# Attention ahead of two expert layers: batch 0's outputs scaled later, strided tokens grouped modulo 8, V loaded in one transfer, idle matmuls around the q and k transposes

## The chip, the cores and the metric

The program runs on one core of a Trainium2 chip. The metric is the device time of one execution in microseconds. TensorE (PE) does matmuls and transposes, VectorE (DVE), ScalarE (ACT) and GpSimd (POOL) do elementwise work, and SyncE (SP) issues the transfers. ACT issues some too. All engines run their own instruction streams and meet only at semaphores.

## What is computed

```
# q, k, v: 4 batches x 8 heads x 576 tokens x 64
scores = q @ k.T / 8
mask_local   = (rel >= 0) & (rel < 32)               # heads 0 to 3
mask_strided = (rel >= 0) & (pos_k % 32 == pos_q % 32)   # heads 4 to 7
attn = softmax(where(mask, scores, -1e9)) @ v        # -> x, 2304 tokens x 512
h = x @ w_in;  g = h * sigmoid(1.702 h);  x = g @ w_out          # d_ff 2048
# top 2 of 8 experts, d_ff 1024, noisy gate
out[token] += weight * (relu(x @ w1[e]) @ w2[e])
```

## The kernel before

**Three stages.** Stage A is the attention, stage B the dense layer with the splitting of the experts' weights beside it, stage D the experts. The change is to stage A and the head of the program, up to about 190 us.

**Stage A.** The eight heads of a batch make four pairs `hp` (0 and 1 local, 2 and 3 strided), so there are 16 pairs `i = 4 b + hp`. The PE program has a prologue (transposes of q and k and the scores of pairs 0 and 1) and then one *body* for each pair. Body `i` holds, in this order: `transpose_p` of head 0 of pair `i`, `transpose_qk` for q and for k of pair `i+2`, `p_times_v` of head 0, `transpose_p` of head 1, `scores` of pair `i+2` head 0, `p_times_v` of head 1, `scores` of pair `i+2` head 1. In the last two bodies the parts of pair `i+2` are replaced by first matmuls of stage B (`mlp_ahead`). Below, T(i) is the time at which the q transposes of body `i` start. The order is written out by hand; nothing is scheduled by a tool.

**Who feeds whom.** `ps_t` (two banks) takes all transposes, and ACT copies them out (`evac_pt`, `evac_qk`). DVE takes row maxima of the scores and subtracts them (`max_and_sub`), ACT takes the exponential (`exps`), DVE sums (`sums`), POOL normalises (`norm`), and PE transposes the result. The output of a pair stands in `ps_o`. ACT writes its scaled fp16 high part (`out_hi`) and DVE the remainder (`out_lo`) into `x1`.

**Scales.** V, w_in, the gate weights and w_out each get one power-of-two factor from their absolute maximum. DVE takes maxima over pieces (`v_max`, `weights_max`, by `absmax`), then the piece results are joined and `raw_max` is counted up. PE spreads the joined column over the partitions by one small matmul that stands at the head of a `scores` (argument `spread`, with a wait on `raw_max`). DVE reduces that (`ALL_OF`), and `power_of_two` makes the factor in five short steps. ACT and DVE then split w_in in eighths in four bodies from `SPLIT_IN`, and w_out from `SPLIT_OUT`.

**Loads.** SP issues them in program order: `load_qk` four transfers with rows of 64 numbers, `load_v` five for a local pair and eight for a strided one, `v_flat` two transfers of 2.3 MB over all of V for its maximum. A strided pair's 576 tokens are treated as 8 groups of 72: with token = 32 j + 4 g + r, group g has the tokens of all j and r.

**Idle matmuls.** `busy` issues matmuls on constants that nobody reads: 12 of 512 columns ahead of the first data, and 4 of 224 columns ahead of each `p_times_v`.

Of the kernel before, what the change touches and what calls it, by code (L numbers as in the profile page):

```python
# [68 lines left out]
MAX_IN, SPLIT_IN, MAX_OUT, SPLIT_OUT = 1, 6, 9, 14  # L69
assert (MAX_IN + QUARTERS) % 4 == 1 and (MAX_OUT + QUARTERS) % 4 == 1  # L70
# [6 lines left out]
def program(nc, q, k, v, w_in, w_out, w_gate, w_noise, noise, w1, w2, out):  # L77
    ctx = ExitStack()
    with ctx:
# [188 lines left out]
        def w2_of(par, part, f):  # L268
# [24 lines left out]
            "consts_pool busy_set qk_in0 qk_in1 v_in0 v_in1 v_in2 v_in3 v_flat_in0 v_flat_in1 w_in_in w_out_in "  # L293
            "small_in t_done t_evac s_done mx_done sub_done exp_done sum_done rr_done norm_done pv_done "
            "x1_hi x1_lo raw_max scaled step split_hi split_lo "
# [18 lines left out]

        def is_local(hp):
            return hp < PAIRS // 2

        V_DMAS = [5, 5, 2 * SRES, 2 * SRES]
# [18 lines left out]
        def out_views(b, hp, part):  # L337

            tok = slice(b * SEQ, (b + 1) * SEQ) if isinstance(b, int) else bass.ds(b * SEQ, SEQ)
            dst = x1[:, part, hp, tok]  # L340
# [48 lines left out]
        def _(sp):  # L389
# [12 lines left out]

            load_qk(0, 0)
            load_qk(0, 1)

            sp.dma_start(w_in_s[:].rearrange("p a c f -> p (a c f)").bitcast(F32)[:, 0:HEADS * SEQ],
                         v[0:2].rearrange("b h (x s) d -> (b h x) (s d)", x=P // (2 * HEADS))
                         ).then_inc(S["v_flat_in0"], 16)
            sp.dma_start(w_out_s[:].rearrange("p a c f -> p (a c f)").bitcast(F32)[:, 0:HEADS * SEQ],
                         v[2:4].rearrange("b h (x s) d -> (b h x) (s d)", x=P // (2 * HEADS))  # L410
                         ).then_inc(S["v_flat_in1"], 16)
            load_v(sp, 0, 0)
            load_v(sp, 0, 1)
# [4 lines left out]
            for i in range(NPAIR - 2):  # L418

                sp.wait_ge(S["s_done"], i * 2 + 2)  # L420
                load_qk((i + 2) // PAIRS, (i + 2) % PAIRS)
                load_v(sp, (i + 2) // PAIRS, (i + 2) % PAIRS)
                if i < QUARTERS:
                    c = DC // QUARTERS
                    wait(sp, S["w_in_in"], 16 * i)
                    sp.dma_start(w_in_raw[:, i * c:(i + 1) * c], w_in.rearrange("(c p) f -> p c f", p=P)[:, i * c:(i + 1) * c]
                                 ).then_inc(S["w_in_in"], 16)
                n, c = i - SPLIT_IN - 3, FC // QUARTERS
# [284 lines left out]
        def _(act):  # L713
            def evac_qk(n, hp, which):
# [26 lines left out]
            def out_hi(b, hp):  # L741
                i = b * PAIRS + hp
                act.wait_ge(S["pv_done"], i * 2 + 2)
                if i == 0:
# [221 lines left out]
        def _(dve):  # L966
# [11 lines left out]
            def power_of_two(src, scale, inverse, link):  # L978
# [11 lines left out]
            v_flat = [t[:].rearrange("p a c f -> p (a c f)").bitcast(F32)[:, 0:HEADS * SEQ]  # L990
                      for t in (w_in_s, w_out_s)]
# [25 lines left out]
            def out_lo(b, hp):  # L1017
                i = b * PAIRS + hp
                dve.wait_ge(S["x1_hi"], i + 1)
                for (src, hi), (_, lo) in zip(out_views(b, hp, 0), out_views(b, hp, 1)):  # L1020
                    last_op = nc.vector.scalar_tensor_tensor(lo, src, col(S_V), hi, ALU.mult, ALU.subtract)  # L1021
                last_op.then_inc(S["x1_lo"], 1)

            def v_max(n):

                half = HEADS * SEQ // 2
                dve.wait_ge(S[f"v_flat_in{n // 2}"], 16)
# [3 lines left out]
            max_and_sub(0, 0, 0)  # L1031
            max_and_sub(0, 0, 1)
            v_max(0)
            sums(0, 0, 0)
            sums(0, 0, 1)
            v_max(1)
            max_and_sub(0, 1, 0)
            max_and_sub(0, 1, 1)
            v_max(2)
# [11 lines left out]
            ALL_OF = {0: V_ALL, 1: WG_ALL, MAX_IN + QUARTERS: WI_ALL, MAX_OUT + QUARTERS: WO_ALL}  # L1051
# [20 lines left out]
            def weights(i):  # L1072

                if i == 0:
                    dve.wait_ge(S["small_in"], 48)
                    nc.vector.tensor_reduce(col(B_MAX), wg[:], AX.XY, ALU.max, apply_absolute_value=True
                                            ).then_inc(S["raw_max"], 1)
                if MAX_IN <= i < MAX_IN + QUARTERS:
                    weights_max(S["w_in_in"], i - MAX_IN)
                if i == SPLIT_IN - 1:  # L1080
                    dve.wait_ge(S["all_max"], 3)
                    power_of_two(col(WI_ALL), col(S_WI), col(I_WI), step).then_inc(S["scaled"], 1)
                if i == 2 * PAIRS:
                    dve.sem_inc(S["raw_max"], 1)
                if MAX_OUT <= i < MAX_OUT + QUARTERS:
                    weights_max(S["w_out_in"], i - MAX_OUT)
# [11 lines left out]
            def stage_a(b, last=False):  # L1098
                for hp in range(PAIRS):
# [7 lines left out]
                    if i == 0:  # L1107
                        v_max(3)
# [767 lines left out]
```

## Time and profile before

| | |
|---|---|
| median of 3 runs | 1030.38 us (1029.64 to 1032.16) |
| the profiled execution | 1028.2 us |
| its span, first to last instruction | 1026.4 us |
| PE busy | 978.1 us (95% of the span) |
| DVE, ACT, POOL busy | 594.5, 307.6, 219.8 us |
| mean granted TensorE clock | 0.976 |

The profile is of one execution, so sums that are made with its rows stand against 1028.2 us; what they give is then put on the median. A busy share is a mean over stages with different limits. "Granted clock" 1.00 is 2.4 GHz and 0.50 is 1.2 GHz.

### The profile page before, as it was taken

What the parts mean: (1) busy time and instruction counts of PE and PEld (TensorE: products, weight loads), DVE (VectorE), ACT (ScalarE), POOL (GpSimd) and SP (SyncE); (2) the same over time, 40 slices, a digit from 0 to 9 for tenths busy, and PEclk for the clock granted to TensorE, in tenths of its full rate; (3) what the DMA queues carried; (4) which work ended last, traced back from release to release, by engine and by line L of the source; (5) the groups of instructions that cost most, each with busy time, mean ns of one, the idle gap of its engine ahead of it and who ended that gap; (6) DMA issues with size and microseconds to landing.
All of it is one profiled execution on the core that took longest, in us unless ns stands there. A gap on an engine that the chain in (4) does not pass through costs nothing.

```text
span 1026.4 us, 22946 instructions
## 1 busy us (share of the span) xinstructions
PE 978.1 (95%) x9218; PEld 706.8 (69%) x9219; DVE 594.5 (58%) x1033; ACT 307.6 (30%) x427; POOL 219.8 (21%) x274
## 2 busy tenths in 40 slices
PE   7899999999999999999999899989999999999992
PEld 4677777867677576775765767756777767677771
DVE  6588998668777786787887744232232323233231
ACT  2355745523243233332531321111111111111110
POOL 4222323000000000010025124233323333333331
PEclk8699999999999999999999999999999999999997
DMA  9774582097756667567647635848474747475330
GB/s 267 177 187 92 129 196 55 6 393 237 249 204 205 247 214 258 181 205 268 219 149 238 218 78 151 263 114 213 131 210 121 221 120 214 133 209 142 89 82 23
DMA packets 170240, 182.43 MB, mean 178 GB/s; under 512 B 133495, under 2 KB 133495, under 8 KB 167360
## 3 DMA queue, kind: packets, MB, share of 16 engines
q1 hardware_dynamic: 112832, 142.47, 44.6%
q0 software_dynamic: 9600, 27.69, 8.9%
q10 hardware_dynamic: 47744, 11.35, 6.3%
q8 instruction: 48, 0.79, 0.3%
q14 instruction: 16, 0.13, 0.0%
HBM read 116.41 MB, written 53.55 MB: 166 GB/s over the span
## 4 chain that ended last, share of the span: by engine, by line
PE 86%; DVE 4%; DMA 2%; SPq 2%; ACT 2%; issue 1%; POOLq 0%; DVEq 0%; ACTq 0%
PE bank L1760 20%; PE bank L1769 20%; PE bank L1661 18%; PE bank L1586 17%; PE bank L1524 4%; PE bank L1562 3%; PE bank L1494 2%; PE bank L1536 1%; PE bank L1543 1%; PE bank L1513 1%; DMA arena<-out,arena 1%; DMA arena<-in_moe_w 1%; DVE sc L976 1%; SPq L399 1%; ACT arena L725 1%
## 5 line engine op out<-in xcount | busy, mean ns | idle before, releaser
L1586 PE MATMUL bank<-x,w_in_s 128*128 128x256 f16 (+1 forms) x1728 | 194.1, 273 | 2.6 <-DVE x L1021 1.5
L1661 PE MATMUL bank<-w_out_s,arena 128*128 128x512 f16 x864 | 190.2, 379 | 0.0
L1586 PEld LDWEIGHTS bank<-x,w_in_s 128*128 128x128 f16 x1728 | 167.9, 98 | 25.9 <-DVE x L1021 1.8
L1661 PEld LDWEIGHTS bank<-w_out_s,arena 128*128 128x128 f16 x864 | 83.6, 98 | 96.6
L1429 DVE TENSOR_TENSOR arena<-arena 128x512 f32<-128x512 f32 x37 | 25.6, 692 | 161.7 <-ACT arena L899 117.6
L1760 PEld LDWEIGHTS bank<-arena,w_out_s 128*128 128x128 f16 x2016 | 114.5, 98 | 5.9 <-issue 0.8
L1760 PE MATMUL bank<-arena,w_out_s 128*128 128x128 f16 x2016 | 117.0, 219 | 0.6 <-issue 0.6
L1760 PEld LDWEIGHTS bank<-arena,w_in_s 128*128 128x128 f16 x1920 | 109.3, 98 | 5.4 <-issue 0.7
L1760 PE MATMUL bank<-arena,w_in_s 128*128 128x128 f16 x1920 | 111.7, 219 | 0.5 <-issue 0.5
L1769 PE MATMUL bank<-w_out_s,arena 128*128 128x512 f16 x480 | 108.7, 383 | 3.3 <-DVE arena L1424 3.3
L1769 PE MATMUL bank<-w_in_s,arena 128*128 128x512 f16 x480 | 108.6, 383 | 2.3 <-DVE arena L1424 2.3
L1422 DVE CAST arena<-arena 128x512 f16<-128x512 f32 x82 | 35.5, 433 | 124.0 <-ACT arena L894 113.2
L976 DVE TENSOR_REDUCE sc<-arena 128x1 f32<-128x512 f32 (+2 forms) x42 | 100.4, 2404 | 7.6 <-DMA arena<-in_moe_w 4.0
L894 ACT ACTIVATE arena<-bank 128x512 f32<-128x512 f32 x82 | 48.9, 597 | 167.4 <-PE bank L1760 152.3
L1158 DVE SCALAR_TENSOR_TENSOR arena<-arena,sc 128x4096 f16<-128x4096 f32 x16 | 71.7, 4483 | 34.7 <-ACT arena L803 34.7
L1769 PEld LDWEIGHTS bank<-w_out_s,arena 128*128 128x128 f16 x480 | 46.5, 99 | 56.7 <-issue 5.9
L1769 PEld LDWEIGHTS bank<-w_in_s,arena 128*128 128x128 f16 x480 | 46.5, 99 | 55.8 <-issue 2.8
L899 ACT ACTIVATE arena<-bank,arena 128x512 f32<-128x512 f32 x40 | 27.5, 687 | 185.9 <-PE bank L1769 182.7
L803 ACT ACTIVATE arena<-arena,sc 128x4096 f16<-128x4096 f32 x16 | 59.3, 3709 | 61.9 <-DVE sc L985 61.9
L632 POOL DMA_INDIRECT arena<-out,arena x37 | 44.2, 1196 | 130.7 <-DMA out<-arena 116.6
L565 POOL TENSOR_TENSOR arena<-arena 96x768 f32<-96x768 f32 (+1 forms) x32 | 44.2, 1397 | 124.8 <-DVE arena L1015 124.7
L637 POOL DMA_INDIRECT out<-arena x40 | 41.4, 1034 | 104.5 <-DVE arena L1429 98.4
(196 smaller groups left out, 992.8 us busy)
## 6 DMA issues: line engine op xcount, KB each, us to landing
arena<-in_moe_w SPq DMA_DIRECT2D x16, 2048.0 KB, 11.5
split_weights<-arena SPq DMA_DIRECT2D x16, 2048.0 KB, 7.4
w_in_s<-split_weights SPq DMA_DIRECT2D x32, 512.0 KB
w_out_s<-split_weights SPq DMA_DIRECT2D x32, 512.0 KB
arena<-in_q SPq DMA_DIRECT2D x32, 144.0 KB, 3.6
arena<-in_k SPq DMA_DIRECT2D x32, 144.0 KB, 3.7
out<-zeros SPq DMA_DIRECT2D x1, 4608.0 KB, 25.1
x_rows<-arena SPq DMA_DIRECT2D x18, 256.0 KB, 3.3
```

The costliest lines, as they stand in the source:

```text
L565: pool.tensor_tensor(pr, pr, rr[hp % 2][0:nq, h2, 0:nb].unsqueeze(2).to_broadcast([nq, nb, nk]), ALU.mult).then_inc(S["norm_done"], 1)
L632: pool.indirect_dma_start(out=prior[b4 % 2], out_offset=None, in_=out, in_offset=bass.IndirectOffsetOnAxis(ap=cur[b4], axis=0), bounds_che ...
L637: pool.indirect_dma_start(out=out, out_offset=bass.IndirectOffsetOnAxis(ap=cur[b4], axis=0), in_=ysb[b4 % 2], in_offset=None, bounds_check ...
L803: nc.scalar.activation(halves[:, 0], raw[m], ACT.Copy, scale=col(S_U + m)).then_inc(S["unit_hi"], 1)
L894: nc.scalar.activation(hf[half], ps_dh[half], ACT.Relu, scale=DOWN).then_inc(S["relu_done"], 1)
L976: return nc.vector.tensor_reduce(dst, src, AX.X, ALU.max, apply_absolute_value=True)
L1158: nc.vector.scalar_tensor_tensor(halves[:, 1], raw[m], col(S_U + m), halves[:, 0], ALU.mult, ALU.subtract).then_inc(S["unit_lo"], 1)
L1524: last = mm(dst, ql, kr, start=False, stop=True, skip_group_check=True)
L1586: last = mm(dst, w_in_s[:, w_part, c, f * P:(f + 1) * P], x1[:, x_part, c, tok], start=(c == 0 and w_part + x_part == 0), stop=(c == DC - ...
L1661: last = mm(ps_x[j], g[par][:, g_part, f, j * P:(j + 1) * P], w_out_s[:, w_part, f], start=(n == 0), stop=(n == 3 * FC - 1))
L1760: last = mm(ps_dh[half][:, n * P:(n + 1) * P], w1_of(w_par, w_part, c, f), xt[par][:, x_part * DC + c], start=(c == 0 and w_part + x_part ...
L1769: last = mm(ps_y[par], h[par][:, h_part, f * P:(f + 1) * P], w2_of(w_par, w_part, f), start=(n == 0), stop=(n == 3 * EFC - 1))
```

## The change

- **Loads.** `load_qk` of pair 2 is issued once the transposes of pair 0 are done, that of pair 3 after those of pair 1. The loads of all of V for its maximum come in four parts of 1.2 MB between them. `load_v` of pairs 0 and 1 is issued by ACT. A strided pair's V comes in one transfer, with rows of 512 numbers.
- **Groups.** token = 8 p + n, group n has all p. So `evac_qk`, the output of `p_times_v` and `out_views` have other access patterns: q and k are written one number at a time with 72 numbers from one to the next, where before four lay side by side; `p_times_v` writes every fourth number of the bank, where before it wrote four side by side out of sixteen.
- **Batch 0's outputs.** ACT copies them unscaled as fp32 into a free part of `x1` (`held_out`). In batch 1 each body has one more scaling on ACT and one more remainder on DVE for them.
- **Maxima.** They move to other bodies. The last pieces of w_in and w_out are now taken inside bodies 6 and 13, ahead of the spreading matmul of the same body (before: at the end of bodies 4 and 12).
- **Idle matmuls.** Two or four of 512 columns between the steps of the prologue, one of 256 columns ahead of each half of `transpose_qk` in the bodies (into a score bank, with a new wait on `sub_done`), and none now ahead of `p_times_v` of head 0.

```diff
-MAX_IN, SPLIT_IN, MAX_OUT, SPLIT_OUT = 1, 6, 9, 14
+SPLIT_IN, SPLIT_OUT = 7, 14
...
+        held_out = [x1[:, 0, hp, 2 * SEQ:4 * SEQ].bitcast(F32) for hp in range(PAIRS)]
...
-        V_DMAS = [5, 5, 2 * SRES, 2 * SRES]
+        V_DMAS = [5, 5, 1, 1]
...
-            dst = dst.rearrange("p (j a x) -> p a j x", j=SLEN, a=2)
-            src = ps_o[:, :, 0:SEQ // 2].rearrange("p a (j x) -> p a j x", j=SLEN)
+            dst = dst.rearrange("p (k a n) -> p a k n", k=SQ, a=2)
+            src = ps_o[:, :, 0:SEQ // 2].rearrange("p a (k n) -> p a k n", k=SQ)
...
-                s = s.rearrange("h (j g r) d -> h r j g d", j=SLEN, g=SB)
-                for h2 in range(2):
-                    for r in range(SRES):
-                        eng.dma_start(vn[hp][r:SQ:SRES, :, h2], s[h2, r]).then_inc(v_in[hp], 16)
+                eng.dma_start(v_tile(hp)[0:SQ].rearrange("p h n d -> p h (n d)"),
+                              s.rearrange("h (p n) d -> p h (n d)", n=SB)).then_inc(v_in[hp], 16)
...
+            sp.wait_ge(S["t_done"], 4)
+            load_qk(0, 2)
+            load_v_flat(0)
+            sp.wait_ge(S["t_done"], 8)
+            load_qk(0, 3)
+            load_v_flat(1)
...
# ACT
-                    dst = dst.rearrange("c (g a j r) -> c a j g r", g=SB, a=2, j=SLEN // 2)
-                    src = src.rearrange("c a (j g r) -> c a j g r", g=SB, r=SRES)
+                    dst = dst.rearrange("c (n a p) -> c a p n", n=SB, a=2)
+                    src = src.rearrange("c a (p n) -> c a p n", n=SB)
...
+                if b == 1:
+                    act.wait_ge(S["x1_lo"], 2 + hp)
+                    nc.scalar.activation(x1[:, 0, hp, 0:SEQ], held_out[hp], ACT.Copy, scale=col(S_V)
+                                         ).then_inc(S["late_hi"], 1)
...
             evac_qk(1, 0, 1)
+            load_v(act, 0, 0)
...
             exps(0, 0, 1)
+            load_v(act, 0, 1)
# DVE
-            ALL_OF = {0: V_ALL, 1: WG_ALL, MAX_IN + QUARTERS: WI_ALL, MAX_OUT + QUARTERS: WO_ALL}
+            ALL_OF = {PAIRS: V_ALL, SPLIT_IN - 1: WI_ALL, 2 * PAIRS + 2: WG_ALL, SPLIT_OUT - 1: WO_ALL}
...
+                    if i == SPLIT_IN - 1:
+                        weights_max(S["w_in_in"], QUARTERS - 1)
+                    if i == SPLIT_OUT - 1:
+                        weights_max(S["w_out_in"], QUARTERS - 1)
                     weights_lo(i, 0)
# PE
+                    busy(idle, slice(0, 2 * P), ps_s[0][:, 0])
                     wait(pe, S["t_evac"], n * 2 + a - 1)
...
-                busy(4, slice(SEQ // 2, 4 * P))
+                if h2 == 1:
+                    busy(4, slice(SEQ // 2, 4 * P))
...
-                        o = o.rearrange("p (j n r) -> p n j r", j=SLEN, n=half)[:, m % half]
+                        o = o.rearrange("p (k n) -> p n k", n=half)[:, m % half]
...
+                    spread = (V_MAX, b + 2) if hp == 0 and not last else (B_MAX, 2 * b + 2) if hp == 2 else None
+                    if hp == 1 and last:
+                        spread = (B_MAX, 7)
...
+                        pe.wait_ge(S["sub_done"], i * 2 + 3)
+                        transpose_qk(k[1], hp2, 0, loads, 1)
+                        transpose_qk(k[2], hp2, 1, loads, 1)
```

The first place is SP's queue at the head of the program, from the load of all of V on. Before, ten transfers of V stand ahead of q and k of pair 2:

```order
L406 DMA w_in_s<-in_v 128x4608
L409 DMA w_out_s<-in_v 128x4608
L351 DMA arena<-in_v 128x2x64
L356 DMA arena<-in_v 32x5x64
L357 DMA arena<-in_v 96x5x64
L356 DMA arena<-in_v 32x5x64
L357 DMA arena<-in_v 96x5x64
L351 DMA arena<-in_v 128x2x64
```

Now pair 2 stands right behind the first eight loads of q and k (here from the third line on), and the V of a strided pair is one row (the last but one):

```order
L402 DMA arena<-in_q 96x6x64 x2
L402 DMA arena<-in_k 96x6x64 x2
L402 DMA arena<-in_q 96x6x64 x2
L402 DMA arena<-in_k 96x6x64 x2
L410 DMA w_in_s<-in_v 128x2304
L402 DMA arena<-in_q 96x6x64 x2
L402 DMA arena<-in_k 96x6x64 x2
L410 DMA w_in_s<-in_v 128x2304
...
L402 DMA arena<-in_k 96x6x64 x2
L366 DMA arena<-in_v 72x2x512 x2
L410 DMA w_out_s<-in_v 128x2304
```

So q and k of pairs 2 and 3 have moved ahead of V, and V's maximum takes its data in between.

The second place is DVE around the last piece of w_in. Before, the piece and the joining of the four results end body 4, and the sums of body 5 and its maxima follow. (`L976` is `absmax`, `L1013` the sums, `L998` the score maxima, `L1000` the reduction of the spread column.)

```order
L976 TENSOR_REDUCE sc<-arena 128x1
L976 TENSOR_REDUCE sc<-sc 128x1
L1013 TENSOR_REDUCE arena<-arena 72x8
L1015 RECIPROCAL arena<-arena 72x8
L1013 TENSOR_REDUCE arena<-arena 72x8
L1015 RECIPROCAL arena<-arena 72x8
L998 TENSOR_REDUCE arena<-bank 72x8
L1000 TENSOR_REDUCE sc<-bank 128x1
```

Now, at the turn from body 5 to body 6 (`L999` is `absmax`, `L1037` the sums, `L1022` the score maxima, `L1024` the reduction of the spread column):

```order
L999 TENSOR_REDUCE sc<-arena 128x1 [waits w_in_in]
L1037 TENSOR_REDUCE arena<-arena 72x8 [waits exp_done]
L1039 RECIPROCAL arena<-arena 72x8 [waits sum_done]
L1037 TENSOR_REDUCE arena<-arena 72x8 [waits exp_done]
L1039 RECIPROCAL arena<-arena 72x8 [waits sum_done]
L999 TENSOR_REDUCE sc<-arena 128x1 [waits w_in_in]
L999 TENSOR_REDUCE sc<-sc 128x1 [waits step]
L1022 TENSOR_REDUCE arena<-bank 96x6 [waits s_done]
L1024 TENSOR_REDUCE sc<-bank 128x1
```

The third piece ends body 5, and the fourth with the joining stands behind the sums of body 6. Body 13 has the same rows for w_out.

## Rows read from the trace of the kernel before

**Rows 1.** The page: granted clock, 40 slices of the span, in tenths.

```profile
PEclk8699999999999999999999999999999999999997
```

**Rows 2.** Timeline of the first 45 us: start, length, engine, line, what [idle before].

```profile
10.32 0.53 PE L1513 MATMUL bank<-arena,identb 96*96 96x384 bf16 x2
12.26 0.71 PE L1494 MATMUL bank<-ident,arena 96*128 96x96 f32 x6
...
28.71 2.46 PE L1494 MATMUL bank<-ident,arena 96*128 96x96 f32 x12 [6.56 <-DMA arena<-in_k]
...
36.40 0.27 PE L1508 MATMUL bank<-identb,sc 128*128 128x128 bf16 x1 [1.21 <-DVE sc L976]
...
40.84 0.14 DVE L980 TENSOR_SCALAR sc<-sc 128x1 f32<-128x1 f32 x1
...
41.59 0.15 DVE L985 TENSOR_SCALAR sc<-sc 128x1 f32<-128x1 f32 x1
...
42.80 1.28 PE L1524 MATMUL bank<-arena 64*72 64x72 f32 x16
...
44.97 0.30 PE L1494 MATMUL bank<-ident,arena 96*128 96x96 f32 x1 [0.25 <-ACT arena L732]
```

**Rows 3.** Timeline of the same stretch, SP's queue.

```profile
11.47 5.91 SPq L351 DMA_DIRECT2D arena<-in_v  x1
...
25.13 1.06 SPq L399 DMA_DIRECT2D arena<-in_k  x2
```

**Rows 4.** Windows of 1 us: PE, PEld, DVE, ACT, POOL busy, granted clock, DMA share, GB/s.

```profile
15.00:16.00 1.00, 1.00 (x8) 0.99 (x8) 1.00 (x1) 0.96 (x2) 0.00 (x0) 0.78 0.90 387
...
42.00:43.00 1.00, 1.00 (x6) 0.40 (x5) 0.00 (x0) 0.72 (x1) 0.00 (x0) 0.56 0.17 38
```

**Rows 5.** Timeline, PE in bodies 7 and 8 (body 8 has body 0's shapes).

```profile
105.79 1.21 PE L1562 MATMUL bank<-arena 72*64 72x72 f32 x16
...
113.90 0.77 PE L1494 MATMUL bank<-ident,arena 96*128 96x96 f32 x6 [0.25 <-ACT arena L732]
114.87 0.77 PE L1494 MATMUL bank<-ident,arena 96*128 96x96 f32 x6 [0.20 <-ACT arena L725]
115.48 0.55 PE L1543 MATMUL bank<-busy_in 128*128 128x224 bf16 x4
115.95 1.21 PE L1562 MATMUL bank<-arena 128*64 128x96 f32 x12
...
117.64 0.22 PE L1508 MATMUL bank<-identb,sc 128*128 128x128 bf16 x1
...
121.22 1.25 PE L1524 MATMUL bank<-arena 64*72 64x72 f32 x16
...
123.37 0.77 PE L1494 MATMUL bank<-ident,arena 96*128 96x96 f32 x6 [0.25 <-ACT arena L732]
```

**Rows 6.** Timeline, end of body 12 and body 13 (starts 162.7 us).

```profile
160.22 0.74 ACT L747 ACTIVATE x<-bank,sc 128x576 f16<-128x576 f32 x1 [2.65 <-PE bank L1562]
...
162.16 0.71 ACT L732 ACTIVATE arena<-bank 128x288 f32<-128x288 f32 x2 [1.21 <-PE bank L1536]
...
163.23 2.27 DVE L976 TENSOR_REDUCE sc<-arena 128x1 f32<-128x2048 f32 x1
...
165.54 0.16 DVE L976 TENSOR_REDUCE sc<-sc 128x1 f32<-128x4 f32 x1
...
166.44 0.22 PE L1508 MATMUL bank<-identb,sc 128*128 128x128 bf16 x1
...
167.24 0.20 DVE L1015 RECIPROCAL arena<-arena 72x8 f32<-72x8 f32 x1
```

**Rows 7.** Timeline of PE behind a wait in stage D.

```profile
670.49 7.03 PE L1769 MATMUL bank<-w_out_s,arena 128*128 128x512 f16 x24 [3.28 <-DVE arena L1424]
```

**Rows 8.** The window of half a microsecond behind it, columns as in rows 4.

```profile
671.00:671.50 0.50, 0.50 (x3) 0.22 (x2) 0.47 (x2) 0.00 (x0) 0.12 (x1) 0.50 0.45 85
```

**Rows 9.** Timeline of the start of stage B, matmuls of 512 columns at full clock.

```profile
208.92 6.64 PE L1661 MATMUL bank<-w_out_s,arena 128*128 128x512 f16 x30
```

More of the change, by code:

```diff
@@ L401, in load_qk, with load_v_flat @@
                                      ).then_inc(qk_in[par], 16)
+            def load_v_flat(n):
+                half = HEADS * SEQ // 2
+                at = slice(n % 2 * half, (n % 2 + 1) * half)
+                rows = v[n // 2 * 2:n // 2 * 2 + 2].rearrange("b h (x s) d -> (b h x) (s d)", x=P // (2 * HEADS))
+                sp.dma_start(v_flat[n // 2][:, at], rows[:, at]).then_inc(S[f"v_flat_in{n}"], 16)
             load_qk(0, 0)
             load_qk(0, 1)
[L406 to L413, printed above, removed]
+            sp.wait_ge(S["t_done"], 4)
[4 more added lines that the diff above has]
+            load_v_flat(1)
             sp.dma_start(wg[:, :, 0:E], w_gate.rearrange("(c p) e -> p c e", p=P)).then_inc(S["small_in"], 16)
@@ L416, in _ @@
             sp.dma_start(noise_sb[:], noise.rearrange("(t p) e -> p t e", p=P)).then_inc(S["small_in"], 16)
-            for i in range(NPAIR - 2):
-                sp.wait_ge(S["s_done"], i * 2 + 2)
+            for i in range(2, NPAIR - 2):
+                sp.wait_ge(S["t_done"], 8 * i - 2)
                 load_qk((i + 2) // PAIRS, (i + 2) % PAIRS)
+                if i == 2:
+                    load_v(sp, 0, 2)
+                    load_v(sp, 0, 3)
+                if i <= 3:
+                    load_v_flat(i)
+                sp.wait_ge(S["pv_done"], 2 * i - 2)
                 load_v(sp, (i + 2) // PAIRS, (i + 2) % PAIRS)
-                if i < QUARTERS:
+                for n in ([0], [1], [2, 3])[i - 2] if i < 5 else []:
                     c = DC // QUARTERS
-                    wait(sp, S["w_in_in"], 16 * i)
-                    sp.dma_start(w_in_raw[:, i * c:(i + 1) * c], w_in.rearrange("(c p) f -> p c f", p=P)[:, i * c:(i + 1) * c]
+                    wait(sp, S["w_in_in"], 16 * n)
+                    sp.dma_start(w_in_raw[:, n * c:(n + 1) * c], w_in.rearrange("(c p) f -> p c f", p=P)[:, n * c:(n + 1) * c]
                                  ).then_inc(S["w_in_in"], 16)
-                n, c = i - SPLIT_IN - 3, FC // QUARTERS
+                n, c = i - SPLIT_IN - 1, FC // QUARTERS
                 if 0 <= n < QUARTERS:
@@ L743, in out_hi @@
                 act.wait_ge(S["pv_done"], i * 2 + 2)
-                if i == 0:
+                if b == 0:
+                    for src, dst in out_views(b, hp, None):
+                        last_op = nc.scalar.activation(dst, src, ACT.Copy)
+                    last_op.then_inc(S["x1_lo"], 1)
+                    return
+                if i == PAIRS:
                     act.wait_ge(S["scaled"], 1)
@@ L1072, in weights @@
             def weights(i):
[L1074 to L1079, printed above, removed]
+                if i < 3:
+                    v_max(i + 1)
+                if i == 2:
+                    dve.wait_ge(S["step"], steps[0])
+                    absmax(col(V_MAX), col(PART_MAX, 4)).then_inc(S["raw_max"], 1)
+                if 3 <= i < SPLIT_IN - 1:
+                    weights_max(S["w_in_in"], i - 3)
+                if i == SPLIT_IN:
+                    gate_max()
                 if i == SPLIT_IN - 1:
-                    dve.wait_ge(S["all_max"], 3)
+                    dve.wait_ge(S["all_max"], 2)
                     power_of_two(col(WI_ALL), col(S_WI), col(I_WI), step).then_inc(S["scaled"], 1)
[L1083 to L1086, printed above, removed]
+                if SPLIT_IN + 3 <= i < SPLIT_OUT - 1:
+                    weights_max(S["w_out_in"], i - SPLIT_IN - 3)
                 if i == SPLIT_OUT - 1:
@@ L1107, in stage_a @@
                     if i == 0:
[L1108 to L1110 removed]
+                        v_max(0)
+                    if i == SPLIT_IN - 1:
+                        weights_max(S["w_in_in"], QUARTERS - 1)
+                    if i == SPLIT_OUT - 1:
+                        weights_max(S["w_out_in"], QUARTERS - 1)
                     weights_lo(i, 0)
@@ L1485, in _, with busy, transpose_qk @@
             mm = nc.tensor.matmul
-            def transpose_qk(n, hp, which, loads):
+            def busy(n, columns=slice(0, 4 * P), ps=ps_busy):
+                for _ in range(n):
+                    mm(ps[:, columns], busy_in[:, 0:P], busy_in[:, P:P + columns.stop - columns.start],
+                       start=True, stop=True, skip_group_check=True)
+            def transpose_qk(n, hp, which, loads, idle=0):
                 pe.wait_ge(qk_in[hp % 2], loads)
@@ L1538, in transpose_p @@
                     last.then_inc(S["t_done"], 1)
-            def busy(n, columns=slice(0, 4 * P)):
-                for _ in range(n):
-                    mm(ps_busy[:, columns], busy_in[:, 0:P], busy_in[:, P:P + columns.stop - columns.start],
-                       start=True, stop=True, skip_group_check=True)
             def p_times_v(n, b, hp, h2, v_use):
@@ L1560, in p_times_v @@
                     else:
-                        o = o.rearrange("p (j n r) -> p n j r", j=SLEN, n=half)[:, m % half]
-                    last = mm(o, vn[hp][0:nk, m, h2], pt[0:nk, m * nq:(m + 1) * nq], start=True, stop=True)
+                        o = o.rearrange("p (k n) -> p n k", n=half)[:, m % half]
+                    values = vn[hp][0:nk, m, h2] if is_local(hp) else v_tile(hp)[0:nk, h2, m]
+                    last = mm(o, values, pt[0:nk, m * nq:(m + 1) * nq], start=True, stop=True)
                 last.then_inc(S["pv_done"], 1)
@@ L1569, in _ @@
             transpose_qk(1, 0, 1, 16 * QK_DMAS)
+            busy(2)
             pe.wait_ge(S["consts_pool"], 10)
             scores(0, 0, 0, 2)
+            busy(2)
             scores(0, 0, 1, 2)
+            busy(2)
             transpose_qk(2, 1, 0, 16 * QK_DMAS)
             transpose_qk(3, 1, 1, 16 * QK_DMAS)
+            busy(2)
             scores(0, 1, 0, 4)
+            busy(2)
             scores(0, 1, 1, 4)
+            busy(4)
             pe.wait_ge(S["consts_pool"], CONSTS)
@@ L1624, in stage_a @@
                     if more:
-                        scores(b2, hp2, 0, k[2] + 1,
-                               (V_MAX, 1) if hp == 0 else (B_MAX, b + 2) if hp == 1 else None)
+                        scores(b2, hp2, 0, k[2] + 1, spread)
                     else:
```

54 lines of the change are left out of this document (29 added, 25 removed).

## The prediction

> **What bounds the kernel now.** I read the page first. TensorE is busy for 95% of the span, and its granted clock is at full nearly everywhere; the exception the change can reach is the dip at the very start [rows 1]. So two questions matter: what PE waits for in the first 45 us, and what it executes or waits for in each body of stage A.
>
> The head, by the timeline: after the prologue and the first transposes of P, PE stands idle for 6.56 us until k of pair 2 has landed, and starts body 0 at 28.71 [rows 2]. The queue of SP tells why: k of pair 2 is issued only at 25.13, since one issue of the transfers of V ahead of it took 5.91 us [rows 3]. The clock had already halved at about 15.5 us and comes back only at about 42.9 [rows 4], so body 0 runs cold and takes 44.97 - 28.71 = 16.26 us [rows 2]. Body 8 has the same shapes and takes 123.37 - 113.90 = 9.47 us at full clock [rows 5].
>
> In the steady bodies PE goes from one piece to the next with only two visible gaps of 0.25 and 0.20 us around the transposes of q and k [rows 5]. DVE also has little air where weights are split, but what ends last is PE.
>
> **The change, part by part.** Gains are negative.
>
> *The head.* Q and k of pair 2 are issued once pair 0 is transposed, some 15 us earlier, so the data is there when PE arrives. What is then the path is PE's own prologue, with idle matmuls added. A group of local scores takes 12.26 - 10.32 = 1.94 us, 512 columns at full clock take 6.64 / 30 = 0.22 us [rows 2, 9]. From the end of the first group at 10.32: 0.43 idle, 1.94 scores, 0.43 idle give 13.1; the twelve transposes with their waits 115.48 - 113.90 = 1.6 [rows 5], then 0.43, 1.94, 0.43, 1.94 and 0.86 give 20.3; the six transposes of P (0.77, as six in rows 5) and the gap of 0.25 give T(0) = 21.4 against 28.71. DVE's sums lose the reduction of V that stood before them, so the normalised P does not delay this. If the clock holds, body 0 takes 9.47 less the 0.41 worked out below, so T(1) = 30.5 against 44.97: **-14.5 us**. It is also the part with the cold body in it, so the clock matters: every window of the new prologue holds 512-column matmuls where the old one had transposes with pauses, and I take it that the clock holds. ACT's own issue of V costs nothing here if its ten issues take about half a microsecond each; they stand ahead of evacuations that PE needs only later.
>
> *Idle matmuls in the bodies.* The four ahead of `p_times_v` of head 0 cost PE 115.95 - 115.48 = 0.47 us [rows 5] and nothing else is waited for there, since P was copied out before the k transposes. The new four of 256 columns take about 0.11 each. Two lie inside the gaps of 0.25 and 0.20; two stand where there is only about 0.05 of gap, and about 0.06 in all comes out behind the last. Bounds: nothing, and all 0.44. So -0.41 in each of bodies 1 to 13, **-5.3 us**, and -0.47 in bodies 14 and 15, which have no q and k: **-0.9 us**.
>
> *The moved wait.* `sub_done` is now needed before the q transposes instead of before the scores. It is for the subtraction of the body before, finished more than a microsecond earlier; nothing, unless DVE is over a microsecond late.
>
> *Batch 0's scaling.* Four copies more on ACT and four remainders more on DVE. Between the start of the output copy and the next evacuation ACT has 162.16 - 160.22 = 1.94 us, of which the copy takes 0.74 [rows 6]; a second of 0.74 fits. In body 4 it does not fit: V's factor is made there, in five steps of 40.84 to 41.74, 0.90 us [rows 2], and `out_hi` waits for them with the evacuation of the next P queued behind it. DVE is also later by a maximum of 2.27 us. **+0.7 us** (0 to 2).
>
> *The last pieces of w_in and w_out.* This is the cost that the change brings. PE's spreading matmul now waits for a maximum that stands behind both sums of the same body. In body 13 of the trace DVE does one piece from 163.23 (2.27 us) and has the sums done at 167.44; PE passes the spread at 166.44 [rows 6]. With the next piece behind the sums: 167.3 + 2.27 + 0.16 [rows 6] and a tenth from there to PE give 169.8, where PE arrives at 166.44 - 0.41 = 166.0. That is 3.8 us of idle PE. DVE comes late into both bodies: in bodies 4 and 5 for the added remainders and pieces, in 10 to 12 because pieces of w_out meet the last eighths of w_in. The bounds are 3.2 (sums limited only by the exponentials) and 5.5; I take 4.5 for each of bodies 6 and 13: **+9.0 us**.
>
> *The clock behind these stalls.* After an idle time of 3.28 us in stage D the clock stood at half [rows 7, 8]. From the spread to the first matmul of the second group of scores a cold body took 42.80 - 36.40 = 6.40 us, a warm one 121.22 - 117.64 = 3.58 [rows 2, 5], and the clock was back right there. So a stall costs another 2.8 us, twice **+5.6 us**. Bounds: nothing, and double, if it stays cold as long as it did from body 0 on.
>
> *Strided groups.* SP has seven issues fewer per strided pair; that queue is hidden behind the bodies. The access patterns are the open point. Sixteen matmuls of 72 columns that write four numbers side by side take 1.21 us, as long as twelve of 96 columns that write plainly [rows 5], so that scatter is free; no row shows single numbers. I take nothing, and up to 1.2 us per head for a doubled write. The Trainium skill speaks against the change here ("SBUF — State Buffer", section "Door 1: The DMA port swizzle"): it says that PSUM has lines of 8 bytes and SBUF of 16, that each new line costs, and that scattered PSUM access slows matmuls clearly. By that rule the old groups of four already paid in PSUM, which the equal 1.21 us speaks against.
>
> *Sum.* -14.5 - 5.3 - 0.9 + 0.7 + 9.0 + 5.6 = -5.4 us. The profiled execution took 1028.2, so 1022.8 for it; the median of the runs shown is 2.2 us above it, so **1025.0 us**.
>
> **The rivals.**
>
> 1. *The stalls stay warm.* One of 3.8 us falls so that the clock holds, or it comes back at once. For it: PE idled 1.21 us ahead of the spread in body 0, and the clock rose 6.5 us later without any change of load. Against it: 3.28 us were enough [rows 7, 8]. Time: 1025.0 - 5.6 = 1019.4.
> 2. *The prologue goes cold as before.* Small fp32 matmuls filled it and still the clock fell at 15.5 with PE almost fully busy [rows 4]. If it also falls now, some 12 us of work at half clock, by the ratio 6.40 to 3.58, take 5.3 us more: 1030.3, no change to be measured.
> 3. *Single-number writes cost.* If `p_times_v` of a strided pair doubles, 16 groups at 1.2 us give +19 and 1044; from 0.52 us per group on (8.5 us in all) the kernel is slower by over 0.3%. The rule of the Trainium skill named above ("SBUF — State Buffer") would have it so. ACT's scattered writes of q and k (a line each, where four shared one) would come on top: the k transposes wait for them.
> 4. *ACT blocks on its issues.* The mechanism is SP's 5.91 us for one issue [rows 3]. ACT issues V of pair 1 between the exponentials and the evacuation of P(0); there the new path has about 1.5 us to spare. One such issue costs 4.4 us and lets the clock fall in the prologue, another 5.3 by rival 2: 1034.7, slower. It decides from 8.5 us on. Against it: the queue of ACT is empty, and SP's first issues of rows just as short did not block.
>
> **How the numbers follow.** A difference of 0.3%, 3.1 us, is about what a measurement here tells from none. My forecast has 0.50, with a range of its own of 1020 to 1030; rival 1 has 0.17, rival 2 0.13, rival 3 0.10, rival 4 0.05, and 0.05 is for others. The forecast's case lies below 1027.3 for 0.36 and above for 0.14; with rival 1 and small parts of the rest faster has 0.60. Rival 2 is mostly "same", which with the forecast's 0.14 makes 0.26, and rivals 3 and 4 leave 0.14 for slower. For the range I go from the warm case with the shorter stalls and the ACT wait at 0 (1019.4 - 1.2 - 0.7 = 1017.5), less another microsecond and a half for shorter prologue work, to the cold head with stalls at 5.5 (1030.3 + 2.0): 1016 to 1032.5.
>
> **What would show it.** In the changed profile T(0) at about 21.4 and T(1) at about 30.5 with the clock at 1.00 throughout; local and strided score bodies 9.1 and 9.7 us apart where 9.47 and 10.1 stood; `absmax` of 2.27 us as what ends PE's idle time ahead of the spread in two places, 4 to 5 us each, and half clock behind both; the matmuls of `p_times_v` of strided pairs still 1.2 us a group. The prediction is wrong if PE idles in the head for longer than 1 us, if the spread finds its maximum ready, or if a strided group takes 1.7 us or more.

## The result, and the profile after

The changed kernel is slower.

| | before | after |
|---|---|---|
| median of 4 runs each, in turn on one chip | 1030.01 us (1024.26 to 1032.16) | 1058.08 us (1052.35 to 1059.53) |
| ratio after to before | | 1.0271 (95% 1.0215 to 1.0327) |
| profiled execution, its span | 1028.2, 1026.4 us | 1058.3, 1056.6 us |
| PE busy | 978.1 us | 1007.1 us |
| mean granted clock | 0.976 | 0.951 |

The ratios here and below compare undisturbed executions alone, the medians are of all. The prediction was 1025.0 us with a range of 1016 to 1032.5; it is wrong in size and in sign. The page already says where to look. PE's work is the same within four instructions, but it is busy 29 us longer, and the row of the granted clock is below full in another place than before:

```profile
PE 1007.1 (95%) x9222; PEld 728.3 (69%) x9224; DVE 593.3 (56%) x1033; ACT 317.9 (30%) x431; POOL 220.7 (21%) x274
...
PEclk9996766899999999999999999999999999999997
```

A slice is 26.4 us. The dip that stood in the first two slices before [rows 1] is gone, and five slices from the fourth to the eighth are low now. Below, "cold" is time at half clock, "warm" is full clock, and a spell is a stretch that stays cold. Windows of 1 us bound the spells: 86 to 121 (34 us of it at half), 137 to 176 (37.5), and two short ones between 188 and 203 us, 81.9 us in all up to 235 us, where the kernel before had 27.3 us, all of them in the head.

The head came out as predicted. PE's timeline of the changed kernel ("after") at the starts of bodies 0 and 1 (T(0) 21.16, T(1) 30.74; before 28.71 and 44.97 [rows 2]), and where the later trouble starts:

```profile
21.16 0.47 PE L1537 MATMUL bank<-ident,arena 96*128 96x96 f32 x3
...
30.74 0.47 PE L1537 MATMUL bank<-ident,arena 96*128 96x96 f32 x3
...
87.63 0.26 PE L1551 MATMUL bank<-identb,sc 128*128 128x128 bf16 x1 [4.25 <-DVE sc L999]
...
116.28 0.74 PE L1537 MATMUL bank<-ident,arena 96*128 96x96 f32 x3
...
137.77 0.40 PE L1526 MATMUL bank<-busy_in 128*128 128x256 bf16 x1 [1.19 <-DMA arena<-in_k]
```

The waits for the spreading matmul are there too: 4.25 us in body 6 and, in body 13, 3.26 us. DVE's timeline of after ahead of the first shows what the prediction had put together from single rows, a piece of 2.27 us, both sums, and the last piece and the joining behind them:

```profile
81.13 2.27 DVE L999 TENSOR_REDUCE sc<-arena 128x1 f32<-128x2048 f32 x1
83.32 0.74 DVE L1037 TENSOR_REDUCE arena<-arena 72x8 f32<-72x576 f32 x1
...
84.22 0.70 DVE L1037 TENSOR_REDUCE arena<-arena 72x8 f32<-72x576 f32 x1
...
85.06 2.23 DVE L999 TENSOR_REDUCE sc<-arena 128x1 f32<-128x2048 f32 x1
87.33 0.16 DVE L999 TENSOR_REDUCE sc<-sc 128x1 f32<-128x4 f32 x1
```

What the prediction did not have stands in these windows of after (us, PE, PEld, DVE, ACT, POOL busy, granted clock, DMA share, GB/s). The clock falls in the wait, and it stays at half for tens of microseconds with PE busy through and through:

```profile
86.00:87.00 1.00, 0.00 (x0) 0.00 (x0) 1.00 (x1) 0.00 (x0) 0.63 (x1) 0.79 0.00 0
104.00:105.00 1.00, 1.00 (x9) 1.00 (x10) 0.97 (x3) 0.44 (x2) 1.00 (x2) 0.50 0.00 0
121.00:122.00 1.00, 1.00 (x12) 0.74 (x10) 0.97 (x3) 1.00 (x2) 0.84 (x1) 1.00 1.03 399
137.00:138.00 1.00, 0.23 (x2) 0.23 (x3) 0.97 (x3) 0.07 (x1) 0.00 (x0) 0.89 1.30 201
138.00:139.00 1.00, 1.00 (x8) 0.99 (x8) 1.00 (x2) 0.32 (x1) 0.00 (x0) 0.50 0.56 91
175.00:176.00 1.00, 1.00 (x11) 0.78 (x10) 1.00 (x2) 1.00 (x3) 0.00 (x0) 0.84 0.00 0
```

Body 7, from T(7) = 99.04 to T(8) = 116.28, takes 17.24 us at half clock; body 3 has the same shapes and takes 9.84 us warm, so 0.43 us are lost per microsecond at half clock. By this estimate 81.9 us of it cost 35.2 us.

The second long spell does not start at a stall that was predicted, but at the wait for k of pair 12 (1.19 us, above). SP's queue in after's timeline tells why k is late, there and for pair 7 in body 5, where PE waited 0.93 us:

```profile
54.62 7.67 SPq L438 DMA_DIRECT2D arena<-in_moe_w_in  x2
62.34 0.98 SPq L402 DMA_DIRECT2D arena<-in_q  x2
...
129.22 0.38 SPq L444 DMA_DIRECT2D arena<-in_moe_w_out  x1
129.65 1.05 SPq L402 DMA_DIRECT2D arena<-in_q  x2
130.74 2.46 SPq L402 DMA_DIRECT2D arena<-in_k  x2
```

What SP's queue waited for, in total, times and longest (us), from after's waits between 40 and 200 us:

```profile
SPq L444 <- DVE w_in_s L1092: 43.5, 4, 23.8
...
SPq L438 <- DMA arena<-in_moe_w_in: 6.9, 1, 6.9
```

The change issues two pieces of w_in in one step. The kernel makes the second wait until the first has landed (`wait(sp, S["w_in_in"], 16 * n)`), so of the row of 7.67 us 6.9 are this wait and the two issues take 0.38 and 0.35; q and k of pair 7 stand behind it. Every piece of w_out is issued one step earlier in the loop than before, while the split comes a body later, so there it waits for DVE's split (`split_lo`) with q and k behind it: the piece at 129.22 was let go 5 us after the piece before it had landed.

The account nearly closes. Behind T(1) after loses 30.2 + 14.2 = 44.4 us against before: 7.5 in the two stalls, 2.1 in waits for k, 35.2 by the clock and 3.2 behind stage A, where it was not followed up, make 48.0. The 3.6 too many are in part what the warm bodies gain; the 0.43 is an estimate from one body.

### The profile page after: what moved, and what is told of

Same layout as the page of the kernel before. It is cut to its first block, busy times and chain, and to the rows that moved or that the text cites. A ratio compares the mean times of both kernels' runs of the same rounds, so it can differ in the third digit from the quotient of the medians.

```text
span 1056.6 us, 22919 instructions
## 1 busy us (share of the span) xinstructions
PE 1007.1 (95%) x9222; PEld 728.3 (69%) x9224; DVE 593.3 (56%) x1033; ACT 317.9 (30%) x431; POOL 220.7 (21%) x274
## 4 chain that ended last, share of the span: by engine, by line
PE 85%; DMA 5%; DVE 3%; ACT 2%; SPq 2%; issue 1%; POOL 1%; ACTq 0%; POOLq 0%; DVEq 0%
PE bank L1808 19%; PE bank L1817 19%; PE bank L1631 18%; PE bank L1709 18%; PE bank L1567 4%; PE bank L1601 3%; PE bank L1537 1%; DMA arena<-in_moe_w_in 1%; DMA arena<-out,arena 1%; PE bank L1526 1%; PE bank L1579 1%; DMA arena<-in_k 1%; PE bank L1556 1%; DMA out<-arena 1%; SPq L402 1%
## 5 line engine op out<-in xcount | busy, mean ns | idle before, releaser
L1631 PEld LDWEIGHTS bank<-x,w_in_s 128*128 128x128 f16 x1728 | 168.4, 98 | 26.4 <-DVE x L1045 1.8
L999 DVE TENSOR_REDUCE sc<-arena 128x1 f32<-128x512 f32 (+2 forms) x42 | 100.3, 2402 | 7.5 <-DMA arena<-in_moe_w 3.9
```

The source lines that it names most:

```text
L999: return nc.vector.tensor_reduce(dst, src, AX.X, ALU.max, apply_absolute_value=True)
L1631: last = mm(dst, w_in_s[:, w_part, c, f * P:(f + 1) * P], x1[:, x_part, c, tok], start=(c == 0 and w_part + x_part == 0), stop=(c == DC - ...
```

## The experiments

Theory A: what drops the clock is PE's idle time in stage A, the stalls and the waits for k, and the bodies' own work brings it back only after tens of microseconds. Theory B, the rival: the clock falls and stays down since the idle matmuls ahead of `p_times_v` of head 0 are gone. Cold time is counted up to 235 us, in the one profiled execution of each kernel. The kernels ran on three chips, the first four against a median of before of 1032.31 us, the next four against 1029.21, the last two against 1029.61; so medians of different groups can differ by 3 us for the chip alone.

**1. All maxima a body earlier, no late pieces.**

```diff
-                    if i == SPLIT_IN - 1:
-                        weights_max(S["w_in_in"], QUARTERS - 1)
-                    if i == SPLIT_OUT - 1:
-                        weights_max(S["w_out_in"], QUARTERS - 1)
...
-                if 3 <= i < SPLIT_IN - 1:
-                    weights_max(S["w_in_in"], i - 3)
+                if i == 2:
+                    dve.wait_ge(S["raw_max"], 3)
+                if 2 <= i < SPLIT_IN - 1:
+                    weights_max(S["w_in_in"], i - 2)
```

(and likewise for w_out)

> The changed kernel with the last pieces of w_in and w_out taken at the end of bodies 5 and 12 again, so that the spread of bodies 6 and 13 finds its maximum (all four pieces one body earlier); everything else as changed. Theory A (a stall drops TensorE's clock, and the bodies' own work brings it back only after tens of us): the 4.25 and 3.26 us stalls and the half clock from 87 to 121 us go, about 4.0 + 3.0 of stall and about 14 of cold work; the second cold spell (138 to 175 us) stays if the 1.2 us wait for k of pair 12 stays. So about 1058 - 21 = 1037, and near 1021 if the second spell goes too. Theory B (the clock falls because the four idle matmuls ahead of head 0 are gone, stalls or not): cold spells remain in bodies 6 to 12, and only the 7 us of stalls are won: about 1051.

Measured: 1036.82 us, ratio 1.0028 (0.9974 to 1.0081). The stalls are gone and 21 of the 28 us with them, but 34 us are cold and PE waits 7.3 us for k in three places. They last 1.72, 2.50 and 3.10 us, and the spells behind them 3.4, 6.8 and 23.9 us. The first one in the timeline:

```profile
71.67 0.27 PE L1524 MATMUL bank<-busy_in 128*128 128x256 bf16 x1 [1.72 <-DMA arena<-in_k]
```

So the late maxima are the larger part of the loss here, and SP's queue looks like the rest.

**2. After, with the idle matmuls ahead of head 0 back.**

```diff
-                if h2 == 1:
-                    busy(4, slice(SEQ // 2, 4 * P))
+                busy(4, slice(SEQ // 2, 4 * P))
```

> The changed kernel with the four idle matmuls of 224 columns ahead of head 0's p_times_v put back, nothing else. Theory A (cold because of stalls): the stalls stay, the cold spells stay as long, and the idle matmuls cost 16 x 0.47 = 7.5 us more at full clock: about 1062 to 1066. Theory B (the removed idle matmuls kept the clock up): the clock returns within about 7 us of each stall, as it did in the head of the kernel before, and some 60 us of half clock at 0.43 us lost per us go: about 1058 - 26 + 8 = 1040.

Measured: 1055.15 us, ratio 1.022 (1.0154 to 1.0287); 41 us cold where after had 82, the stalls (6.7 us) and the waits for k (5.6 us) still there. The time lies between what the two theories had. In the one trace the cold time is half, but it does not go, the longer waits and the matmuls' own time eat most of the gain, and the time hardly moves. B may explain a part of how long a spell lasts, not its start.

**3. Before, with the last pieces behind the sums of bodies 5 and 13.**

```diff
-                if MAX_IN <= i < MAX_IN + QUARTERS:
+                if MAX_IN <= i < MAX_IN + QUARTERS - 1:
...
                         sums(b1, hp1, 1)
+                    if i == MAX_IN + QUARTERS:
+                        weights_max(S["w_in_in"], QUARTERS - 1)
```

(and likewise for w_out)

> The kernel before with only the place of the last pieces changed: those of w_in and w_out are taken in bodies 5 and 13 behind the sums and ahead of the spread, as the change has them. Theory A: two stalls of 3 to 4 us and behind the first one a cold spell of tens of us, as in the changed kernel: 1030 + 7 of stalls + 3 to 14 of cold for each: 1045 to 1060. Theory B: with the old idle matmuls the clock falls at most for 6.5 us behind each stall: 1030 + 7 + 5.6 = 1043 or less, with no spell over 7 us.

Measured: 1060.38 us, ratio 1.0244 (1.0139 to 1.0349): the moved maxima alone cost about what the whole change does. Cold are 96 us, 48 of them in one spell from 96 to 144 us, with the idle matmuls of before all in place, behind a wait for the spread of only 2.5 us. This is against B. The head, which the edit does not touch, was cold for 37.6 us here against 27.3 in before's trace, so some 4 us of the difference are not the edit's. Behind the second wait, 2.54 us, the spell was 6.8 us.

**4. The maxima earlier (1) and the loads in another order.** One piece of w_in per step, w_out a step later.

```diff
-                for n in ([0], [1], [2, 3])[i - 2] if i < 5 else []:
+                for n in [i - 2] if i < 6 else []:
...
-                n, c = i - SPLIT_IN - 1, FC // QUARTERS
+                n, c = i - SPLIT_IN - 2, FC // QUARTERS
```

> e1_early_max and besides the transfers of w_in (last piece) and w_out one step later in SP's queue, so that they no longer stand ahead of q and k of the next pair while they wait for a split. Theory A: no wait for k at bodies 5 and 10, no stall, no cold spell in bodies 1 to 12: stage A as warm as before and the head's 14.5 us kept, less about 0.3 us per local body for the idle matmuls: about 1030 - 14.2 - 2.5 = 1013. Theory B: cold spells remain without any wait: above 1030.

Measured: 1015.58 us, ratio 0.986 (0.9779 to 0.9941); 3.4 us cold, and no wait for a transfer. The predicted wait for V's factor is visible now: ACT's scaled copy waits for the last step of the factor, batch 0's scaling (L768) follows, and PE waits at the start of body 5 for the copy of P queued behind both:

```profile
69.83 0.74 ACT L764 ACTIVATE x<-bank,sc 128x576 f16<-128x576 f32 x1 [3.61 <-DVE sc L1008]
...
70.47 0.77 ACT L768 ACTIVATE x<-x,sc 128x576 f16<-128x576 f32 x1
...
71.59 0.47 PE L1535 MATMUL bank<-ident,arena 96*128 96x96 f32 x3 [0.62 <-ACT arena L744]
```

**5. After, with the load order of (4) only.**

> The changed kernel with only the queue mended: the last piece of w_in and the pieces of w_out are issued one step later by SP. The late maxima stay. Theory A (idle time of PE drops the clock, the bodies do not bring it back quickly): the waits for k of about 1 us at bodies 5 and 10 go, and with the second of them what started the spell of 138 to 175 us; the 4.2 and 3.3 us stalls stay with the spell behind the first. 1058 - 2 - 16 = about 1040, between 1030 and 1048. If the spell of 138 us had nothing to do with the wait for k, it stays and the time is 1055.

Measured: 1038.11 us, ratio 1.0068 (1.0029 to 1.0107); stalls of 7.5 us, no wait for k, 23.9 us cold. With (1) and (4) this makes a square of medians: late maxima and old order 1058.1, early maxima 1036.8, new order 1038.1, both 1015.6. By these each is worth 20 to 22.5 us, by the ratios (1.0271, 1.0028, 1.0068, 0.986) 17 to 25. They add up as far as intervals of 4 to 8 us to either side can tell. The wait for the spread in body 6 is 4.24 us here as in after, but in this trace only 17 us are cold behind it and not 34.

**6. (5) with work in the stalls.** Ahead of the spread of bodies 6 and 13 PE executes 36 idle matmuls, 3.62 us. The wait remains; only what PE does in it changes. PE's loop over batches is unrolled for it.

```diff
+                    if i in (6, 13):
+                        busy(36, slice(SEQ // 2, 4 * P))
                     if more:
                         scores(b2, hp2, 0, k[2] + 1, spread)
```

> e5_loads with 36 idle matmuls of 224 columns (4.3 us at full clock) ahead of the spread in bodies 6 and 13, where PE stands idle, and with PE's loop over the batches written out so that they stand in these two bodies only. PE then reaches the spread about as late as its maximum is ready, and is as late as in e5_loads, but never idle. Theory A: the clock stays at 1.00 behind both, so stage A costs what e4_early_max_loads costs and 2 x 4 us: 1015.6 + 8 = about 1023 to 1025. A rival, that the spell comes of DVE's or ACT's lateness behind the stall and not of PE's idle time, has no gain: as e5_loads, about 1040.

Measured: 1022.0 us, ratio 0.9928 (0.9895 to 0.9961), 6.8 us cold. PE's timeline around the spread of body 6 in kernel 5, then in kernel 6:

```profile
82.90 0.69 PE L1579 MATMUL bank<-ident,arena 72*72 72x72 f32 x8
87.83 0.27 PE L1551 MATMUL bank<-identb,sc 128*128 128x128 bf16 x1 [4.24 <-DVE sc L999]
87.90 0.84 PE L1556 MATMUL bank<-arena,identb 96*96 96x384 bf16 x2
```

```profile
86.57 0.69 PE L1579 MATMUL bank<-ident,arena 72*72 72x72 f32 x8
87.10 3.62 PE L1526 MATMUL bank<-busy_in 128*128 128x224 bf16 x36
91.50 0.22 PE L1551 MATMUL bank<-identb,sc 128*128 128x128 bf16 x1 [0.79 <-DVE sc L999]
91.56 0.49 PE L1556 MATMUL bank<-arena,identb 96*96 96x384 bf16 x2
```

The spread passes no earlier in its body, but the matmuls behind it take 0.49 us for two instead of 0.84. Between the medians lie 16 us, by the ratios 14. The two profiled executions are 6.7 us apart with 17.1 us fewer cold, 7.3 by the estimate of 0.43; kernel 5's was one of its faster ones, since its mean granted clock went from 0.963 to 0.980 over its executions and kernel 6's from 0.986 to 0.993. The unrolling is no rival: warm bodies take the same in both to 0.01 us, such as 9.58, 9.50 and 9.87. So in these two places PE's idle time is what drops the clock, and the drop costs more than the wait.

**7. (4) with ACT's copy of strided q and k turned round.** It reads its bank with a step of 8 numbers and writes side by side.

```diff
-                    dst = dst.rearrange("c (n a p) -> c a p n", n=SB, a=2)
-                    src = src.rearrange("c a (p n) -> c a p n", n=SB)
+                    dst = dst.rearrange("c (n a p) -> c a n p", n=SB, a=2)
+                    src = src.rearrange("c a (p n) -> c a n p", n=SB)
```

> e4_early_max_loads with ACT's copy of q and k of strided pairs walked the other way round: it reads PSUM at every eighth number and writes 36 numbers side by side, where it read side by side and wrote single numbers 72 apart. If scattered writes are what makes the copy 0.69 instead of 0.41 us, it is 0.41 now, the second gap at the k transposes is 0.1 instead of 0.30 us, and seven bodies gain 0.3 us: 1015.6 - 2 = 1013.6. If scattered PSUM reads cost as much, no change: 1015.6; if more, up to 1020.

Measured: 1017.05 us, ratio 0.985 (0.979 to 0.991). The bodies that transpose strided q and k take 9.05 and 9.14 us instead of 9.50 and 9.57, but neither medians nor ratios can tell the kernel from (4). ACT's copies, from the groups by shape of the first 200 us (busy us, mean ns of one), in after and then in kernel 10, which has this edit:

```profile
L737 ACT ACTIVATE arena<-bank 128x288 f32<-128x288 f32 x64 | 31.7, 558 | 16.9 <-PE bank L1537 16.8
```

```profile
L737 ACT ACTIVATE arena<-bank 128x288 f32<-128x288 f32 x64 | 23.5, 405 | 15.3 <-PE bank L1535 15.3
```

**8. (4) with the idle matmuls ahead of head 0 back** (edit as in 2).

> e4_early_max_loads with the four idle matmuls ahead of head 0 put back. At full clock they cost what the prediction said, 0.47 us in each of 16 bodies: 1015.6 + 7.5 = 1023.1. If they were partly hidden, less; if they kept a clock up that e4_early_max_loads lets fall in some executions, the spread of the times gets smaller and the median comes out lower than 1023.

Measured: 1020.81 us, ratio 0.9936 (0.9903 to 0.997), nothing cold at all. Where the clock holds without them, these matmuls cost 0.39 us in every warm body (9.96 us for 9.57, 10.25 for 9.86), where the prediction had 0.47 from the row. The kernel is slower than (4) by 5.2 us by the medians and by 8 by the ratios, with intervals too wide to say more.

**9 and 10. (7) without the idle matmuls between the q and k transposes, and (7) again beside it.**

```diff
-                        transpose_qk(k[1], hp2, 0, loads, 1)
-                        transpose_qk(k[2], hp2, 1, loads, 1)
+                        transpose_qk(k[1], hp2, 0, loads)
+                        transpose_qk(k[2], hp2, 1, loads)
```

> The same kernel as the one with all maxima a body earlier, the load order changed and ACT's copy of strided q and k reading its bank at stride 8. It is timed beside the next one and for an interval of its own. Theory A (the clock in stage A decides, and it holds when PE nowhere waits for over a microsecond): about 1016 us again, ratio 0.985, granted clock 0.99. Theory B: no difference to A, since this kernel has no idle matmuls ahead of head 0 either.

> The kernel of the run beside it, without the four idle matmuls of 256 columns between the transposes of q and k of each body. What they cost PE was taken as 0.06 us per body in the prediction; the traces gave -0.3 in all for bodies where -0.41 was predicted, so some 0.15 per body. Theory A (what drops the clock is idle time of PE, and gaps of 0.2 us are none): the clock holds, and the time falls by 14 times 0.05 to 0.2, 1 to 3 us: 1014 us. Theory B (the clock needs the idle columns to stay up): half clock appears in bodies that wait for nothing, 0.43 us are lost per cold microsecond, and the time is above the run beside it by 3 us or more.

Measured: 1013.04 us, ratio 0.9844 (0.9802 to 0.9887) with them, and 1028.92 us, 0.9942 (0.9901 to 0.9983) without. Theory A had 1014 for the latter and falls as it stood. Warm bodies take 9.08, 8.99 and 9.81 us without and 9.14, 9.05 and 9.87 us with them, so they cost 0.06 us per body; but without them 61.5 us are cold against 3.4. By the ratios they are worth 10 us, by the medians 15.9. PE's timeline of kernel 9 where the second spell begins, and the windows of the same place:

```profile
85.18 0.69 PE L1577 MATMUL bank<-ident,arena 72*72 72x72 f32 x8
86.12 0.77 PE L1535 MATMUL bank<-ident,arena 96*128 96x96 f32 x6 [0.25 <-ACT arena L744]
87.08 1.22 PE L1535 MATMUL bank<-ident,arena 96*128 96x96 f32 x6 [0.20 <-ACT arena L737]
```

```profile
85.00:86.00 1.00, 0.87 (x12) 0.63 (x10) 1.00 (x3) 0.48 (x3) 0.00 (x0) 1.00 0.46 104
86.00:87.00 1.00, 0.77 (x6) 0.57 (x6) 0.97 (x3) 0.74 (x4) 0.00 (x0) 1.00 0.62 143
87.00:88.00 1.00, 0.92 (x6) 0.92 (x6) 1.00 (x2) 1.00 (x4) 0.00 (x0) 0.53 0.55 126
```

No wait here is longer than 0.25 us, and the clock still falls at 87 us and is back only at 124. The first spell of this kernel, from 59 to 81 us, stands behind waits of 0.31 and 0.73 us. At T(13) kernel 9 is 20 us behind kernel 10; 14.6 us remain in the spans. What replaces theory A: a wait can drop the clock, and in this work short gaps between transposes can do it too; the idle matmuls between them cost next to nothing and mostly hold it. Body 2 of the same kernel had the same gaps and stayed warm, so which gaps do it stays open. So does how long a spell lasts: behind waits of 2.9 to 4.3 us there were 3.4 (kernel 5, second stall) to 34 us (after) at half clock, and no run varied that alone.

## Why the prediction was wrong

*The head: right.* -14.5 predicted, -14.2 measured at T(1); T(0) 21.16 for 21.4, T(1) 30.74 for 30.5, clock at full throughout. ACT did not block on its issues, and the prologue did not go cold, so rivals 2 and 4 are out.

*The last pieces: right in kind, the size a little over.* 4.25 + 3.26 = 7.5 us for 9.0. The prediction's own working gave 3.8 for one; it took 4.5.

*The clock behind these stalls: the step that failed.* The mechanism was named, but sized with "the clock was back right there": 6.5 us at half clock, 2.8 us per stall, at most twice that. It was taken from the end of a cold spell in body 0 [rows 2, 4], so it measured the rest of a spell and not a whole one. After the first stall 34.1 us were cold, after the second 6.8. At 0.43 these 40.9 us are 17.6 us of time where the sum had 5.6; the spell of 37.5 us behind a wait for k, 16.1 us more, had no term at all, and all cold time together makes the 35.2. Before's own trace held a better reading: it was cold from 15.5 to 42.9 us, and PE worked for most of it. Kernels 5 and 6 show the term directly, 14 to 16 us for two stalls with the loads in order.

*"That queue is hidden behind the bodies": the second step that failed.* It counted the issues that went away, and not that pieces of w_in and w_out now wait in SP's queue ahead of q and k. The waits themselves are only 0.93 and 1.19 us, but at the second a spell of 37.5 us begins, and without the stalls they are 7.3 us and, with the cold behind them, cost 21 us by the medians of kernels 1 and 4 (17 by the ratios).

*Idle matmuls: right one by one, and the gain did not come.* Their price in the turnings is the 0.06 us per body that was taken (kernels 9 and 10), and those taken away are worth 0.39 us per body for 0.47 (kernel 8). Bodies with local q and k gained the 0.3 us that this leaves, but those with strided ones lost 0.06 to 0.11, for ACT's copies cost them 0.45 (next point). With the waits in some of them, bodies 1 to 12 took 117.9 us in warm kernel 4 and 117.7 before, where the prediction had some 4 us less. It also priced the matmuls by PE's time alone; that those in the turnings hold up the clock, 10 to 16 us by kernels 9 and 10, no term had. The "local" bodies of its last paragraph (9.47 us before) are those whose own pair is local; the q, k and scores that they make are of strided pairs.

*Strided groups: rival 3 falls for PE, a part holds for ACT.* Sixteen matmuls of a strided group still take 1.21 to 1.22 us. Reading a bank with a step of 8 numbers costs nothing either (0.405 us per copy on average, as before with 0.404). ACT's writes of single numbers cost: 0.56 us is the mean of both kinds, and those of strided pairs alone take 0.67 to 0.75. The sum had nothing for them; in the bodies it is the 0.45 us by which kernel 7 is shorter. The rule of the Trainium skill ("SBUF — State Buffer", section "Door 1: The DMA port swizzle") that scattered PSUM access slows matmuls clearly is not borne out here; its other half, that each new line in SBUF costs, agrees with ACT's 0.7 against 0.41 us.

*Batch 0's scaling: right.* 0.7 predicted, 0.62 us of wait in kernel 4, where nothing else covers it, and 1.07 in kernel 10. The moved wait on `sub_done` is next to it: 0.60 us in body 4 of kernel 10, where nothing was predicted.

None of the four rivals was what happened. The sum without the two stalls and the clock behind them, -5.4 - 9.0 - 5.6 = -20.0 us, is near what kernel 4 gives, where stalls and waits for k are taken away: -16.7 us by the medians. That is in part luck, since the head gives nearly all of it and the 5.3 us for the idle matmuls are not there.

## What to carry to other kernels

Where PE's clock can fall, price a wait by the spell that follows it and not by its own length: here 17 and 34 us at half clock followed the same 4.25 us of idle time in two kernels, 7 to 15 us of time. One profiled execution does not show how long spells get; compare the mean granted clock over several. Read the length of a whole spell, from its start to its end, in a trace of work of the same kind. When loads are reordered, write the queue out step by step and look at which small, urgent transfer now stands behind a large one that waits for something, since a microsecond there can start such a spell. And before an idle matmul is removed as waste, find out by a run whether the clock needs it: of two kinds here one cost 0.39 us in every body, the other was worth 10 to 16 us in all.

## What was not expected of the hardware

- The clock stayed at half for 34 to 48 us of fp32 transposes and small matmuls with PE busy nearly without a gap (windows of after, kernel 3), where the prediction took 6.5.
- Waits of 1.0 to 2.5 us stood ahead of a fall (kernel 6, after, kernel 3), though waits of 0.93 us (after) and 1.10 us (kernel 8) did not bring one, and in kernel 9 none longer than 0.25 us, in a window in which PE was busy for 0.77 of the time.
- 36 idle matmuls of 224 columns (3.62 us) in place of a wait kept it at full there; the two such places were worth 14 to 16 us.
- The same wait of 4.24 and 4.25 us was followed by 17 us at half clock in kernel 5 and 34 in after.
- ACT writes 128 x 288 single fp32 numbers, each 72 numbers from the last, in about 0.7 us, and takes 0.41 us when it reads scattered and writes side by side.
